# A new order of the first six steps, chunk 7 routed like the others, later transposes, and an unrolled ring of expert blocks

## The chip, the cores and the metric

The kernel runs on one core of a Trainium2 chip. The metric is the device time of one execution in microseconds; lower is better. Inputs and outputs are float32 in the chip's memory.

## The reference

Windowed attention, a two-layer network with a Mish activation, and a layer of eight experts with a skip decision for each token. Cut to what matters:

```python
attn_out = _attn_ref(q, k, v)                # 4 batches, 8 heads, 576 positions, head width 64; a query sees
                                             # the 64 positions up to its own; softmax with scale 1/8
x = attn_out.transpose(0, 2, 1, 3).reshape(2304, 512)
h = x @ w_in                                 # w_in 512 x 2048
sp = np.log1p(np.exp(np.minimum(h, 20.0)))   # h itself where h > 20
x = (h * np.tanh(sp)) @ w_out                # w_out 2048 x 512
do_compute = x @ w_skip > 0
xc = x[do_compute]
logits = xc @ w_gate                         # 8 experts
e_idx = np.argmax(logits, axis=1)
gate_w = softmax(logits)[chosen expert]
for e in range(8):                           # w1[e] 512 x 1024, w2[e] 1024 x 512
    y[e_idx == e] = gate_w * (np.maximum(xc @ w1[e], 0.0) @ w2[e])
out[do_compute] = xc + y                     # the other rows are x itself
```

## The kernel before

**Chunks and steps.** The 2304 tokens are worked in NC = 9 chunks of 256: 64 positions of each of the 4 batches. Within a chunk the hidden width 2048 is worked in NJ = 8 steps of 256 columns. Step J = 8c + j is one call of `tick(J)` on each engine. TensorE (PE) does `up(J+2)` in it, 24 matmuls that make the hidden values two steps ahead, and `down_hi(J)` and `down_lo(J)`, 8 and 4 matmuls that add step J's product to the two tiles of y. Values are split into a rounded part and a rest (hi and lo) so that three fast matmuls stand for one of full precision; the first four steps (RAW = 4) use the unsplit product instead, `down_raw`, in 8 matmuls of float32. Mish takes, for each step, on ScalarE (ACT) `mish_exp` (L977) and `mish_recip` (L984, L986), on VectorE (DVE) `mish_n` (L1252, L1257) and `mish_a`, `mish_b`, `mish_c` (L1266, L1272, L1285), on GpSimd (POOL) `mish_q` (L1701); then ACT rounds the product (`g_hi_out`, L992) and POOL takes the rest (`g_lo_out`, L1707).

**Attention** of the next chunk runs between the steps, one group of one batch for every two steps: `scores` (L606, in the steady state L627), `soften` on DVE (mask and maximum), `att_exp` on ACT, `normalise` on DVE, `probs_T` (L635), `probs_T_out` on ACT, `weigh_v` (L648), `x_hi_out` on ACT, `x_lo_out` on DVE (L1245). Chunk 0 has its own forms, `scores_first` to `x_lo_out_first` (L1201), ahead of all steps, with small dummy matmuls (`keep_warm`, L596) between them.

**Weights.** The 16 slices of the two matrices come in 512 KB loads issued by SyncE (SP, L429). Each is rounded by POOL or ACT (`round_slice`, L946 on ACT) and its rest is taken by DVE (`rest_of_slice`, L1209), in the orders HI_POOL, HI_ACT and LO_DVE. `load_group(g)` waits until the attention group two before it has been weighed, and everything behind it on SP's queue waits with it.

**Routing** of chunk c-1 is done in the steps of chunk c. y is transposed in two tiles (`y_T`, L750, copied out by ACT, L1006). For chunks 0 to 6 the logits are made in columns (`logits_columns`, L662, in step j = 2, copied by ACT, then `logits_back`, L672, in j = 4, summed by DVE, L1302); for chunks 7 and 8 they are made by rows (`logits`, L760, 8 matmuls for each tile; DVE copies them out, L1296). Then DVE's `choose` and `gate_and_row`, and a scatter by POOL. For chunk 7 these steps come one j later than for the others (`route_at`).

**Early experts.** DVE's `pick_first` (L1371 and on) at the end of step 63 and `pick_second` at the end of step 64 choose the two fullest experts from the counts of chunks 0 to 6, so that SP can load their weights (2 MB each, L476, L480) and POOL their tokens during chunk 8.

**Expert blocks.** 128 tokens of one expert are a block: `expert_up` (L822, 64 matmuls) and `expert_down` (L840, 24). Blocks 0 to 7 are written out. From block 8 on every engine runs a loop, `Fori(2, 7)`, whose body holds RING = 4 blocks, each inside an `If` on the number of blocks `nblk`, nested, so that the first false `If` skips the rest of the body. The inputs give 12 blocks, 8 to 11 in the loop's first turn. After the last block POOL scatters the rows, DVE waits for that and does one tiny instruction, and the engines meet at the end (L55).

**What sets the order.** Each engine works its own list in order; semaphores tie them. Up to step 5 (OPENING = 6) the lists of PE, ACT and DVE are written out by hand, afterwards `tick` makes them.

## Time and profile before

| | us |
|---|---|
| median of 3 runs | 689.06 (688.34 to 690.7) |
| the profiled execution | 690.12 |
| its span, first to last instruction | 688.5 |
| PE busy | 665.6 (97%), 5192 matmuls |
| DVE, ACT, POOL busy | 486.4, 360.3, 254.3 |

Waits are idle time of an engine just before an instruction, put down to what released it. A line number is that of the kernel's line or of its helper. Matmuls overlap: one of 512 columns is shown as 0.39 us long, but the next starts 0.23 us after it, so that stretches from start to start tell more than durations.

### The profile page before, as it was taken

Reading aid. Unit: us, or ns where it says so; the run is one execution under the profiler, and the core shown is the slowest. Engines: PE = TensorE matmul, PEld = TensorE weight load, DVE = VectorE, ACT = ScalarE, POOL = GpSimd, SP = SyncE. Lnnn points to the kernel's source line nnn. Section 1 sums busy time; section 2 is a strip of 40 time slices with the busy share of each in tenths; the row PEclk is TensorE's granted clock in tenths of the full one; section 3 lists DMA queues with packets and bytes.
Section 4 is the critical chain, followed back from the end, with each engine's and each line's share of the span. In section 5 each row is a group of like instructions: output and inputs, shape, how many; then the busy total and the mean of one; then the engine's idle time right before and its main releaser. Section 6 shows DMA issues by size and latency. Waiting matters only on the chain.

```text
span 688.5 us, 14197 instructions
## 1 busy us (share of the span) xinstructions
PE 665.6 (97%) x5192; PEld 581.0 (84%) x5192; DVE 486.4 (71%) x961; ACT 360.3 (52%) x791; POOL 254.3 (37%) x231
## 2 busy tenths in 40 slices
PE   7798999999999999999999999999999999999994
PEld 6676888888888888888888888888888998999994
DVE  5896777876777795786696687689589754464461
ACT  5545576555664565556556556644453243533530
POOL 4411343443352444353343345345553332221221
PEclk9999999999999999999999999999999999999998
DMA  9815131162156222134115115002658899999940
GB/s 281 276 58 164 40 95 53 39 93 62 63 92 109 77 57 83 45 88 87 40 46 132 39 40 126 14 19 45 245 167 258 258 397 393 370 340 354 354 148 2
DMA packets 62948, 97.20 MB, mean 141 GB/s; under 512 B 23126, under 2 KB 27222, under 8 KB 62880
## 3 DMA queue, kind: packets, MB, share of 16 engines
q1 hardware_dynamic: 59264, 91.01, 43.5%
q0 software_dynamic: 3168, 4.51, 2.1%
q8 instruction: 41, 0.67, 0.4%
q10 hardware_dynamic: 448, 0.79, 0.4%
q14 instruction: 27, 0.22, 0.1%
HBM read 84.97 MB, written 13.73 MB: 143 GB/s over the span
## 4 chain that ended last, share of the span: by engine, by line
PE 80%; DVE 10%; issue 4%; DMA 3%; ACT 3%; SPq 0%; DVEq 0%; POOLq 0%; ACTq 0%
PE Y L715 24%; PE H L687 16%; PE H L822 11%; PE OB L840 10%; PE PTB L687 8%; PE OB L648 3%; PE SB_ L627 2%; PE SB_ L635 2%; PE Y L729 1%; DVE a_sb L1272 1%; DVE a_sb L1266 1%; DVE g_sb L1285 1%; DVE u_sb L1252 1%; DMA wout<-moe_w_out 1%; DMA xs<-y_rows,blk_tok 1%
## 5 line engine op out<-in xcount | busy, mean ns | idle before, releaser
L1701 POOL TENSOR_TENSOR q_sb<-n_sb,r_sb 128x512 f32<-128x512 f32 x72 | 94.0, 1306 | 270.6 <-ACT r_sb L986 155.9
L715 PE MATMUL Y<-wout_hi,g_hi 128*128 128x512 f32 x272 | 111.3, 409 | 3.4 <-ACT g_hi L992 3.1
L687 PE MATMUL H<-x_hi,win_hi 128*128 128x256 f32 x384 | 111.3, 290 | 0.6 <-DVE x_lo L1201 0.5
L687 PE MATMUL H<-x_hi,win_lo 128*128 128x256 f32 x384 | 108.0, 281 | 0.0
L687 PE MATMUL H<-x_lo,win_hi 128*128 128x256 f32 x384 | 107.9, 281 | 0.0
L715 PE MATMUL Y<-wout_lo,g_hi 128*128 128x512 f32 x272 | 107.5, 395 | 0.0
L1707 POOL TENSOR_TENSOR g_lo<-g_sb,g_hi 128x512 fp32r<-128x512 f32 x68 | 88.2, 1296 | 2.4 <-ACT g_hi L992 1.9
L822 PEld LDWEIGHTS H<-xT,w 128*128 128x128 f32 x768 | 87.6, 192 | 1.0
L822 PE MATMUL H<-xT,w 128*128 128x128 f32 x768 | 88.0, 276 | 0.0
L1252 DVE TENSOR_SCALAR u_sb<-e_sb 128x512 f32<-128x512 f32 x72 | 36.5, 508 | 62.3 <-ACT e_sb L977 61.6
L687 PEld LDWEIGHTS H<-x_hi,win_hi 128*128 128x128 f32 x384 | 72.3, 188 | 5.2 <-issue 2.9
L715 PE MATMUL Y<-wout_hi,g_lo 128*128 128x512 f32 x272 | 75.1, 398 | 0.0
L992 ACT CAST g_hi<-g_sb 128x512 fp32r<-128x512 f32 x68 | 42.0, 618 | 60.6 <-DVE g_sb L1285 60.6
L687 PEld LDWEIGHTS H<-x_lo,win_hi 128*128 128x128 f32 x384 | 72.5, 189 | 1.0 <-issue 0.2
L687 PEld LDWEIGHTS H<-x_hi,win_lo 128*128 128x128 f32 x384 | 72.4, 189 | 0.0
L984 ACT ACTIVATE r_sb<-n_sb,two 128x512 f32<-128x512 f32 x72 | 52.1, 723 | 30.8 <-DVE n_sb L1257 30.4
L715 PEld LDWEIGHTS Y<-wout_hi,g_hi 128*128 128x128 f32 x272 | 51.2, 188 | 15.0 <-ACT g_hi L992 5.2
L715 PEld LDWEIGHTS Y<-wout_hi,g_lo 128*128 128x128 f32 x272 | 50.3, 188 | 11.8 <-POOL g_lo L1707 0.3
L715 PEld LDWEIGHTS Y<-wout_lo,g_hi 128*128 128x128 f32 x272 | 51.2, 188 | 9.2
L1037 ACT CAST w_hi<-w 128x1024 fp32r<-128x1024 f32 x44 | 43.1, 1045 | 24.7 <-DMA w<-moe_w 24.7
L687 PE MATMUL PTB<-x_hi,win_hi 128*128 128x256 f32 x192 | 55.4, 288 | 0.0
L1433 DVE TENSOR_TENSOR w_lo<-w,w_hi 128x1024 fp32r<-128x1024 f32 x44 | 51.4, 1223 | 4.1 <-ACT w_hi L1037 4.0
(219 smaller groups left out, 1397.8 us busy)
## 6 DMA issues: line engine op xcount, KB each, us to landing
w<-moe_w SPq DMA_DIRECT2D x23, 2048.0 KB, 10.2
kT<-k_T SPq DMA_DIRECT2D x32, 256.0 KB, 3.3
vw<-v_w SPq DMA_DIRECT2D x32, 256.0 KB, 3.2
y_rows<-ytile SPq DMA_DIRECT2D x36, 128.2 KB, 7.5
out_rows<-ytile SPq DMA_DIRECT2D x36, 128.0 KB, 2.6
win<-moe_w_in SPq DMA_DIRECT2D x8, 512.0 KB, 8.6
qbd<-q_T SPq DMA_DIRECT2D x64, 64.0 KB, 2.6
wout<-moe_w_out SPq DMA_DIRECT2D x8, 512.0 KB, 8.3
```

What stands on the lines that cost most here:

```text
L648: last = nc.tensor.matmul(OB[hp, r * W:(r + 1) * W], vw[:, b % 2, r * P + h * 64:r * P + h * 64 + 64], pT[:, i, half * 64:half * 64 + 64], ...
L687: last = nc.tensor.matmul(HM3[J % 3][:, f, :], wt[:, j, d, f * P:(f + 1) * P], xt[:, c % 2, d, :], start=(n == 0), stop=(n == 3 * DB - 1))
L715: last = nc.tensor.matmul(Y[t][:, :], gt[:, J % 2, lo:lo + P], wt[:, 2 * j + f, :], start=(j == 0 and f == 0 and wt is wout_hi and gt is g ...
L822: last = nc.tensor.matmul(H[half][:, f * P:(f + 1) * P], w1[:, par, o:o + P], xT[:, par, d, :], start=(d == 0), stop=(d == DB - 1))
L840: last = nc.tensor.matmul(OB[:, :], hT[:, f, :], wt, start=first[0], stop=(f == EFB - 1 and hT is hT_lo))
L984: nc.scalar.activation(r_sb[:, J % 2, :], n_sb[:, J % 2, :], ACT.Ln, bias=two[:, 0:1]).then_inc(t_ok, 1)
L992: nc.scalar.copy(g_hi[:, J % 2, :], g_sb[:, :]).then_inc(ghi_ok, 1)
L1037: nc.scalar.copy(w2_hi[par][:, k * 1024:(k + 1) * 1024], w2_raw(b, slot_)[:, k * 1024:(k + 1) * 1024])\
L1252: nc.vector.tensor_scalar(u_sb[:, :], e_sb[:, :], EXP10, 2.0, ALU.min, ALU.add).then_inc(u_ok, 1)
L1433: nc.vector.tensor_tensor(w2_rest(b, slot_)[:, at], w2_raw(b, slot_)[:, at], w2_hi[par][:, at].bitcast(FP32), ALU.subtract)\
L1701: nc.gpsimd.tensor_tensor(q_sb[:, :], n_sb[:, J % 2, :], r_sb[:, J % 2, :], ALU.mult).then_inc(q_ok, 1)
L1707: nc.gpsimd.tensor_tensor(g_lo[:, J % 2, :], g_sb[:, :], g_hi[:, J % 2, :].bitcast(FP32), ALU.subtract)\
```

## The change

It does five things. (1) The hand-written lists of PE, ACT and DVE up to step 5 get another order, the order of slices in LO_DVE changes a little, and PE does 36 dummy matmuls at the start in place of 28. (2) On SP, two slices go ahead of the load of attention group 6 and the last four ahead of that of group 7. (3) Chunk 7 is routed in columns like chunks 0 to 6, at the same j as they, its `logits_back` in j = 3 of chunk 8; in j = 2 there is no `weigh_v` in front of `logits_columns`. (4) For all chunks up to 7 the transposition of y's second tile moves from between `down_hi` and `down_lo` of j = 1 to behind `probs_T` of j = 2, ahead of `down_hi`, and its copy on ACT from before `g_hi_out` to behind `probs_T_out`. `pick_first`, `pick_second` and POOL's `early_tokens` each come one step later. (5) The loop over the expert blocks is written out for blocks 8 to 27 on all engines, nested `If`s on `nblk > b` with constants for b.

```diff
@@ -293,7 +293,7 @@
         HI_POOL = (0, 2, 4, 6, 8)
         HI_ACT = (10, 12, 14, 9, 11, 13, 15, 1, 3, 5, 7)
-        LO_DVE = (0, 2, 4, 6, 8, 12, 14, 10, 9, 11, 13, 15, 1, 3, 5, 7)
+        LO_DVE = (0, 2, 4, 6, 8, 12, 14, 10, 11, 13, 9, 15, 1, 3, 5, 7)
         RAW = 4
         OPENING = 6
         QUAD = 2 * NB + 1
@@ -324,16 +324,17 @@
         def route_at(c, j):
-            return None if c == 0 else j - 1 if c == NC - 1 else j
-
-        def in_columns(c):
-
-            return c < NC - 2
+            return None if c == 0 else j
         def columns_at(J):
             c, j = divmod(J, NJ)
-            return c - 1 if c > 0 and j == 2 and in_columns(c - 1) else None
+            return c - 1 if c > 0 and j == 2 else None
+
+        def back_at(J):
+
+            c, j = divmod(J, NJ)
+            return c - 1 if c > 0 and j == (3 if c == NC - 1 else 4) else None
         def x_at(J):
@@ -343,11 +344,10 @@
             for b in range(2, NE):
                 block_of(b, b // RING, b % RING)
-            with eng.Fori(NE // RING, LOOPS) as i:
-                with ExitStack() as guards:
-                    for n in range(RING):
-                        guards.enter_context(eng.If(i * RING + n < nblk))
-                        block_of(i * RING + n, i, n)
+            with ExitStack() as guards:
+                for b in range(NE, NBLK):
+                    guards.enter_context(eng.If(nblk > b))
+                    block_of(b, b // RING, b % RING)
         def third(b):
@@ -444,12 +444,12 @@
             load_group(5, 1)
             for s in (8, 3, 10, 5, 12):
                 load_slice(s)
-            load_group(6, 0)
             for s in (7, 14):
                 load_slice(s)
-            load_group(7, 1)
+            load_group(6, 0)
             for s in (9, 11, 13, 15):
                 load_slice(s)
+            load_group(7, 1)
             sp.wait_ge(consts, 2)
             sp.dma_start(wrt[:, :, 0:NE + 1], w_rt.rearrange("(d p) n -> p d n", p=P)).then_inc(wrt_in, 16)
@@ -544,11 +544,10 @@
             nblk = sp.value_load(cbi_i[0:1, NV - 1:NV], min_val=NE, max_val=NBLK)
             for b in range(EARLY + 1, NE):
                 load_block(b, b // RING, b % RING)
-            with sp.Fori(NE // RING, LOOPS) as i:
-                with ExitStack() as guards:
-                    for n in range(RING):
-                        guards.enter_context(sp.If(i * RING + n < nblk))
-                        load_block(i * RING + n, i, n)
+            with ExitStack() as guards:
+                for b in range(NE, NBLK):
+                    guards.enter_context(sp.If(nblk > b))
+                    load_block(b, b // RING, b % RING)
             sp.wait_ge(y_out[0], 128 * 6)
             sp.wait_ge(y_out[1], 128 * 5)
@@ -739,10 +738,7 @@
                 elif final:
                     pe.wait_ge(y1_ok, 1)
                 elif not final:
-                    if in_columns(c):
-                        pe.wait_ge(yT_ok, c * 2 + 1)
-                    else:
-                        pe.wait_ge(lg_ok, c * 2 + 1)
+                    pe.wait_ge(yT_ok, c * 2 + 1)
                     beside = scores_at((c + 1) * NJ + 1)
                     if beside:
                         pe.wait_ge(masked_ok, masked(beside[0] * 4 + beside[1]))
@@ -785,20 +781,16 @@
                 if gp:
                     probs_T(*gp)
                 route = route_at(c, j)
-                if route == 0:
-                    y_T(c - 1, 0)
-                if route == 2 and not in_columns(c - 1):
-                    logits(c - 1, 1)
-                if route == 4 and in_columns(c - 1):
-                    logits_back(c - 1)
+                if route in (0, 2):
+                    y_T(c - 1, route // 2)
+                if back_at(J) is not None:
+                    logits_back(back_at(J))
                 down_hi(J)
-                if route == 0 and not in_columns(c - 1):
-                    logits(c - 1, 0)
-                if route == 1:
-                    y_T(c - 1, 1)
                 down_lo(J)
                 if gp:
                     weigh_v(*gp, columns_at(J))
+                elif columns_at(J) is not None:
+                    logits_columns(columns_at(J)).then_inc(pv_ok, 1)
                 if c > 0 and j == 5:
                     ranks(c - 1)
@@ -844,7 +836,7 @@
                     last.then_inc(bz_ok, 1)
             pe.wait_ge(ones_ok, 1)
-            keep_warm(28)
+            keep_warm(36)
             scores_first(0)
             scores_first(1)
             scores_first(2)
@@ -859,35 +851,37 @@
             keep_warm(4)
             weigh_v_first(1)
             probs_T_first(3)
+            scores(1, 0)
             weigh_v_first(2)
             weigh_v_first(3)
-            scores(1, 0)
             up(0)
             up(1)
             probs_T(1, 0)
+            up(2)
             weigh_v(1, 0)
             scores(1, 1)
-            up(2)
             down_raw(0)
+            up(3)
             probs_T(1, 1)
-            up(3)
-            scores(1, 2)
             down_raw(1)
             weigh_v(1, 1)
+            scores(1, 2)
             up(4)
+            down_raw(2)
             probs_T(1, 2)
             up(5)
             weigh_v(1, 2)
-            down_raw(2)
+            up(6)
             scores(1, 3)
             down_raw(3)
-            up(6)
+            up(7)
             probs_T(1, 3)
-            up(7)
+            down_hi(4)
             scores(2, 0)
-            down(4)
             weigh_v(1, 3)
-            down(5)
+            down_lo(4)
+            down_hi(5)
+            down_lo(5)
             for J in range(OPENING, NC * NJ):
                 tick(J)
             rows_T(1, 0, 1)
@@ -1055,18 +1049,16 @@
                 if gx:
                     x_hi_out(*gx)
                 if columns_at(J - 1) is not None:
-                    logits_columns_out(columns_at(J - 1), gx[0] * 4 + gx[1])
+                    logits_columns_out(columns_at(J - 1), gx[0] * 4 + gx[1] if gx else NG)
                 if ahead:
                     mish_recip(J + 1)
                 if c > 0 and j == 0:
                     y_out_of_psum(c - 1)
-                if route_at(c, j) == 2:
-                    y_T_out(c - 1, 1)
                 g_hi_out(J)
                 if gp:
                     probs_T_out(*gp)
-                if route_at(c, j) == 0:
-                    y_T_out(c - 1, 0)
+                if route_at(c, j) in (0, 2):
+                    y_T_out(c - 1, j // 2)
                 if c > 0 and j == 4:
                     route_exp(c - 1)
                 if late_slice(J):
@@ -1093,8 +1085,8 @@
             exp_first(2)
             probs_T_out_first(0)
             exp_first(3)
+            x_hi_out_first(0)
             probs_T_out_first(1)
-            x_hi_out_first(0)
             probs_T_out_first(2)
             x_hi_out_first(1)
             probs_T_out_first(3)
@@ -1106,31 +1098,31 @@
             probs_T_out(1, 0)
             mish_exp(1)
             round_slice(10)
+            mish_recip(1)
             x_hi_out(1, 0)
-            mish_recip(1)
             round_slice(12)
             att_exp(1, 1)
             mish_exp(2)
             round_slice(14)
+            round_slice(9)
+            mish_recip(2)
+            round_slice(11)
+            mish_exp(3)
+            round_slice(13)
             probs_T_out(1, 1)
-            mish_recip(2)
-            mish_exp(3)
+            mish_recip(3)
+            x_hi_out(1, 1)
+            round_slice(15)
             att_exp(1, 2)
-            x_hi_out(1, 1)
-            mish_recip(3)
             mish_exp(4)
+            mish_recip(4)
             probs_T_out(1, 2)
-            round_slice(9)
-            round_slice(11)
             mish_exp(5)
-            mish_recip(4)
-            round_slice(13)
-            round_slice(15)
             x_hi_out(1, 2)
+            mish_exp(6)
+            mish_recip(5)
             att_exp(1, 3)
-            mish_recip(5)
             g_hi_out(4)
-            mish_exp(6)
             probs_T_out(1, 3)
             mish_recip(6)
             g_hi_out(5)
@@ -1460,12 +1452,10 @@
                     mish_n(J + 1)
                 if gp:
                     normalise(*gp)
+                if c == NC - 1 and j == 4:
+                    logits_back_out(c - 1)
                 mish_g(J)
-                if route_at(c, j) == 0 and not in_columns(c - 1):
-                    logits_out(c - 1, 0)
-                if route_at(c, j) == 2 and not in_columns(c - 1):
-                    logits_out(c - 1, 1)
-                if route_at(c, j) == 4 and in_columns(c - 1):
+                if back_at(J) is not None and c < NC - 1:
                     logits_back_out(c - 1)
                 if gx:
                     x_lo_out(*gx, columns_at(J - 1))
@@ -1479,9 +1469,9 @@
                     step, count = steps(rstep, (c - 1) * RSTEPS + 8)
                     gate_and_row(c - 1, step)
                     assert count[0] == RSTEPS - 7, count
-                if c == NC - 2 and j == 7:
+                if c == NC - 1 and j == 0:
                     pick_first()
-                if c == NC - 1 and j == 0:
+                if c == NC - 1 and j == 1:
                     pick_second()
                 if c == NC - 1 and j in (3, 5):
                     rest_of_w2(0, 0, j - 3)
@@ -1503,61 +1493,61 @@
             normalise_first(1)
             soften_first(3)
             normalise_first(2)
+            normalise_first(3)
             rest_of_slice(0)
-            normalise_first(3)
             x_lo_out_first(0)
             x_lo_out_first(1)
+            soften(1, 0)
             x_lo_out_first(2)
+            x_lo_out_first(3)
             rest_of_slice(2)
-            x_lo_out_first(3)
-            soften(1, 0)
+            normalise(1, 0)
             rest_of_slice(4)
             dve.wait_ge(consts, 2)
             mish_n(0)
-            normalise(1, 0)
             rest_of_slice(6)
-            rest_of_slice(8)
             mish_a(0)
             mish_n(1)
+            mish_b(0)
+            mish_c(0)
             soften(1, 1)
-            mish_b(0)
-            x_lo_out(1, 0)
-            mish_c(0)
+            rest_of_slice(8)
             mish_a(1)
-            rest_of_slice(12)
             normalise(1, 1)
             mish_b(1)
             mish_n(2)
+            x_lo_out(1, 0)
             mish_c(1)
+            rest_of_slice(12)
             rest_of_slice(14)
+            mish_n(3)
             mish_a(2)
             rest_of_slice(10)
             soften(1, 2)
             mish_b(2)
-            mish_n(3)
+            x_lo_out(1, 1)
             mish_c(2)
-            x_lo_out(1, 1)
             normalise(1, 2)
+            mish_n(4)
+            rest_of_slice(11)
+            rest_of_slice(13)
             mish_a(3)
-            mish_n(4)
             mish_b(3)
+            mish_c(3)
+            mish_a(4)
+            mish_b(4)
+            x_lo_out(1, 2)
+            mish_n(5)
             rest_of_slice(9)
-            rest_of_slice(11)
-            mish_c(3)
-            rest_of_slice(13)
-            x_lo_out(1, 2)
             soften(1, 3)
-            mish_a(4)
-            mish_n(5)
-            mish_b(4)
-            normalise(1, 3)
             mish_c(4)
             mish_a(5)
+            mish_b(5)
+            normalise(1, 3)
             mish_n(6)
-            mish_b(5)
             rest_of_slice(15)
+            mish_c(5)
             soften(2, 0)
-            mish_c(5)
             x_lo_out(1, 3)
             for J in range(OPENING, NC * NJ):
                 tick(J)
@@ -1759,7 +1749,7 @@
                     all_placed(c - 1)
                 if c == 1 and j == 1:
                     nc.gpsimd.memset(blank[:, :], 0.0).then_inc(blank_ok, 1)
-                if c == NC - 1 and j == 1:
+                if c == NC - 1 and j == 2:
                     early_tokens()
                 if c == NC - 1 and j == 3:
                     pool.wait_ge(g2_ok, J)
```

## Rows read from the trace of the kernel before

**Rows 1.** Page, part 1: busy time, share of the span, instructions

```profile
PE 665.6 (97%) x5192; PEld 581.0 (84%) x5192; DVE 486.4 (71%) x961; ACT 360.3 (52%) x791; POOL 254.3 (37%) x231
```

**Rows 2.** Busy time by stage: stretch, PE, PEld, DVE, ACT, POOL, clock, DMA

```profile
0.00:19.01 19.01, 14.40 (x213) 12.53 (x213) 11.13 (x31) 10.29 (x41) 8.33 (x24) 1.00 0.94 285
19.01:78.33 59.32, 53.72 (x361) 41.64 (x361) 49.26 (x73) 33.51 (x80) 15.48 (x13) 0.97 0.44 138
...
470.00:533.90 63.90, 61.17 (x394) 53.81 (x393) 51.23 (x123) 30.54 (x48) 28.52 (x27) 1.00 0.57 190
```

**Rows 3.** PE's waits over the span: total, times, longest

```profile
PE Y L729 <- DVE g_raw L1285: 3.2, 2, 1.9
PE Y L715 <- ACT g_hi L992: 3.1, 5, 1.4
```

**Rows 4.** Same view as Rows 2, of single pieces of PE's list

```profile
39.24:42.16 2.92, 2.92 (x27) 2.92 (x26) 1.68 (x3) 1.84 (x3) 0.69 (x1) 1.00 0.02 6
42.16:43.05 0.89, 0.89 (x11) 0.89 (x9) 0.89 (x1) 0.60 (x1) 0.89 (x1) 1.00 0.00 0
43.05:46.58 3.53, 3.53 (x11) 1.34 (x9) 3.50 (x5) 0.89 (x5) 0.20 (x1) 1.00 0.00 0
46.58:47.19 0.61, 0.61 (x17) 0.54 (x16) 0.58 (x2) 0.61 (x4) 0.00 (x0) 1.00 0.00 0
50.13:50.49 0.36, 0.36 (x7) 0.36 (x5) 0.36 (x1) 0.16 (x1) 0.28 (x1) 1.00 0.56 155
75.43:78.33 2.90, 2.90 (x13) 2.36 (x13) 2.31 (x6) 2.89 (x11) 1.29 (x1) 1.00 0.36 58
```

**Rows 5.** Instructions of PE in order of time, opening: start, length, idle before

```profile
33.66 5.39 PE L729 MATMUL Y<-wout,g_raw 128*128 128x512 f32 x8 [1.92 <-DVE g_raw L1285]
...
59.98 0.70 PE L729 MATMUL Y<-wout,g_raw 128*128 128x512 f32 x1 [1.27 <-DVE g_raw L1285]
```

**Rows 6.** The same of SP and of ACT

```profile
49.66 2.04 SPq L429 DMA_DIRECT2D wout<-moe_w_out  x4
...
55.67 1.04 ACT L946 CAST wout_hi<-wout 128x1024 fp32r<-128x1024 f32 x1 [4.26 <-DMA wout<-moe_w_out]
```

**Rows 7.** The same of DVE

```profile
17.38 1.24 DVE L1209 TENSOR_TENSOR win_lo<-win,win_hi 128x1024 fp32r<-128x1024 f32 x1
```

**Rows 8.** DVE's groups from 19 to 78.3: busy, mean ns, idle before

```profile
L1209 DVE TENSOR_TENSOR win_lo<-win,win_hi 128x1024 fp32r<-128x1024 f32 x6 | 9.4, 1576 | 0.0
...
L1209 DVE TENSOR_TENSOR wout_lo<-wout,wout_hi 128x1024 fp32r<-128x1024 f32 x4 | 5.1, 1284 | 5.0 <-ACT wout_hi L946 4.9
```

**Rows 9.** Instructions of PE in chunk 4, in order of time

```profile
268.81 1.17 PE L715 MATMUL Y<-wout_hi,g_lo 128*128 128x512 f32 x4
...
274.95 1.09 PE L715 MATMUL Y<-wout_hi,g_lo 128*128 128x512 f32 x4
```

**Rows 10.** Instructions of DVE and PE around chunk 8's start

```profile
467.58 2.79 DVE L1371 TENSOR_TENSOR df<-nextrow,ecap 128x8 f32<-128x8 f32 x1
...
475.87 0.50 PE L715 MATMUL Y<-wout_hi,g_hi 128*128 128x512 f32 x1 [1.43 <-ACT g_hi L992]
...
484.89 0.17 DVE L1296 COPY lg<-MB 128x9 f32<-128x9 f32 x1 [3.84 <-PE MB L760]
...
496.06 0.17 DVE L1296 COPY lg<-MB 128x9 f32<-128x9 f32 x1 [2.79 <-PE MB L760]
```

**Rows 11.** Logits by rows and in columns on PE

```profile
276.58 0.64 PE L662 MATMUL OB<-yT,wrt 128*32 128x256 f32 x8
...
483.90 0.96 PE L760 MATMUL MB<-wrt,yT 128*128 128x9 f32 x8
```

**Rows 12.** The end: chain piece (start, length), then POOL's sequencer lines (ns)

```profile
681.57 2.27 DMA out_rows<-ot,blk_tok
...
L55 POOLq DRAIN  x1: 4971/4971/4971, 683.3 to 683.3; - x1
...
L346 POOLq COMPARE_BRANCH  x5: 48/53/63, 681.4 to 683.3; - x5
```

## The prediction, made before the change was run

> **What bounds the kernel now.** I read the page's busy times first: PE is busy 97% of the span [rows 1]. DVE's 71% is an average, so I cut the span into stages. From the first `up` at 19.01 to the end of step 5's product at 78.33 PE is busy 53.72 of 59.32 us and DVE 49.26; in chunk 8 and after it, 470 to 533.9, PE is busy 61.17 of 63.90 [rows 2]. The stages between are full. So the time lies in three places only: the opening, chunk 8, and what comes after the last matmul. PE's own waits name the releasers: 3.2 us for `g_raw` in two waits and 3.1 us for `g_hi` in five [rows 3]. Elsewhere only PE's own work counts, and it changes only where matmuls are dropped or stand in another company.
>
> **The opening (part 1 and 2).** First PE's floor. One `up` takes 2.92 us, `scores` 0.89, `down_raw` 3.53, `weigh_v` 0.61, `probs_T` 0.36, a split `down` 2.90 [rows 4]. From the first `up` on, the new list holds 8 `up` (23.4), 4 `scores` (3.6), 4 `down_raw` (14.1), 4 `weigh_v` (2.4), 4 `probs_T` (1.4; I take 1.6, as the first one behind an `up` starts slowly) and 2 `down` (5.8): 50.9 us. The stretch took 59.32, so 8.4 us of it are not PE's work: 1.92 and 1.27 us stood before two `down_raw`, and behind the first of these PE ran 5.39 us for what takes 3.60 [rows 5]; the clock of this stage averages 0.97, and 0.03 of 59.3 us is the same 1.8 us: one piece ran at 1.2 GHz in place of 2.4 after PE had idled, and goes back to full rate if the idling goes.
>
> Then what made DVE late. ACT waited 4.26 us for slice 9, because SP issued the last four slices at 49.66, behind the load of group 7 [rows 6]; DVE waited 4.9 us for the rounded slices in turn [rows 8]. The change issues them ahead of that load, behind group 6's, so about 18 us earlier: this idle time goes. What is late next is DVE itself. Its busy time in the stretch, 49.26, less the 2.31 behind the last product that PE needs [rows 4], less the softening of group 4 that moves in front (about 1.4, half of a step's Mish; estimate), plus slice 2's split of 1.24 that moves in [rows 7], is 46.8. Its idle time, 59.32 - 49.26 = 10.1, less 4.9, is 5.2.
>
> The start. PE does 8 more dummies; 28 of them take some 3.3 us, so the first scores come 0.8 us later, and the chain of the first chunk behind them too. On DVE two `x_lo_out_first` now stand behind the softening of group 4, so `up(0)` starts no sooner: I take 19.7. What pays is that the softening and ACT's exponentials of group 4 are ready about 1.3 us earlier.
>
> So by PE alone the stretch ends at 19.7 + 50.9 = 70.6 (gain 7.7). By DVE it ends at 19.7 + 46.8 + 5.2, plus the last 2.9 us that are PE's: 74.6 (gain 3.7). Going through the new lists instruction by instruction with the durations of the old ones I find PE waiting some 0.9, 0.3 and 1.8 us ahead of the first three raw products, none long enough to be sure that the clock falls again, and the end at 73.6 (gain 4.7). I take 4.5. The bounds: 7.7, and 1.0 if DVE is held more often. This needs a word: six slices' splits took 1576 ns on average where 1240 is what one takes alone [rows 7, 8], since a DVE instruction with two SBUF inputs that meets a POOL operation lasts until that one is over. Such holds are 6 us of DVE's 49.26. Their number depends on which instructions meet, which I can't foresee.
>
> **The early steps of chunk 1.** The late slices are rounded there, and `g_hi` is just late in j = 2. ACT's copy of y's second tile leaves the front of that `g_hi_out`, but DVE was the later one: 0.2 us (0 to 0.6).
>
> **The transposition (part 4).** In chunk 4 `down_lo` behind a transposition took 1.17 us, behind other products 1.09 [rows 9]. Moved next to `probs_T`, where the switch to transposes is paid anyway, it costs PE nothing more and saves that 0.08: 7 chunks, 0.6 us. It adds 0.36 us before `down_hi` of j = 2, but PE comes there 0.4 us earlier. The copy on ACT now delays the next `mish_exp` by some 0.1 us; the `g_hi` of j = 3 had 1.0 us to spare, so nothing (if that cover is gone, 0.1 a chunk). Bounds 0 and 0.7.
>
> **Chunk 8 (parts 3 and 4).** The first small instruction of `pick_first`, on 8 columns, took 2.79 us, held by two POOL operations in a row. `mish_n(65)` was queued behind it, then ACT's reciprocal, the copies of y and `g_hi(64)`: PE waited 1.43 us [rows 10]. Without it `g_hi(64)` comes 1.1 to 1.4 us earlier, and y's own copy ends about when PE arrives: this stop goes. The picks now sit in the slack of steps 64 and 65. I expect each to be held once by a `mish_q` or `g_lo_out` (1.3 us each) and PE to wait about 0.45 us behind each: 0.9 back. The logits by rows go: two times 8 matmuls of 0.96 us as shown, against one of 0.64 and a short way back [rows 11], about 0.9 us of PE's time. With them go two waits of DVE, 3.84 and 2.79 us, for PE's logits [rows 10]. But in j = 3 ACT now waits for the columns, then rounds expert weights, and DVE takes their rests before it turns to `mish_n(69)`: PE waits there about 1.1 us instead of 0.56. From j = 5 on the ACT and DVE chain is the bound, not PE, so what PE's list lost is not earned in full. Step 70's `down_hi` I find at 514.5 in place of 515.9: 1.4 us gained. Bounds 0 and 3.3 (all waits for `g_hi`). Choosing later delays SP's load of expert weights and POOL's of tokens by 2 to 6 us: the tokens are gathered 13 us later, but the first weight load ends about when ACT wants it; if it is late, 1 us, inside these bounds.
>
> **The unrolled ring (part 5).** The blocks themselves are PE-bound and keep their 13.1 us each. Behind the last scatter POOL makes five turns through the loop's branches, 681.4 to 683.3, and only then its DRAIN, 4.97 us long, ends the span; the scatter's own transfer had landed 2.27 us after its start, at 683.8 [rows 12]. If the drain takes 4.97 us from its start, 1.9 us are to be had; if it waits for something behind the landing, nothing. A branch now leads over 16 written-out blocks, to code that may have to be fetched; the nearest price is a trip to memory and back such as those 2.27 us: the tail can then lie 0.4 us later than before. I take 0.4 us gained, between 1.9 gained and 0.4 lost.
> The Trainium skill, page "Runtime: NRT & Kernel Launch", section "Instruction fetch mechanics", says that a taken branch whose target is outside the two pages at hand stalls for a fetch. By this rule the one long branch costs and the four short ones it replaces did not, which is the lost end; the trace of before has no such long branch on POOL, so it can't show it.
>
> **The sum.** 4.5 + 0.2 + 0.6 + 1.4 + 0.4 = 7.1 us off the profiled 690.12 (span 688.5, 1.6 around it), 683.0. The profiled execution lay 1.06 above the median of 689.06: 682.0.
>
> **The rivals.**
> A. DVE stays the bound of the opening: its holds and waits are those of before but for the late slices, and chunk 8 gives nothing. For it speaks that DVE is busy 83% of the stretch, and that a searched order is as fragile as its durations. Gain 2 to 4: about 686.
> B. The lists go through without a stop, the picks find gaps, the drain moves: 7.7 + 0.6 + 0.6 + 3.3 + 1.9 = 14 at most; some 11 is plausible: 678.
> C. Nothing to measure: the opening's gain is lost to its later start and one more spell at half clock (1.8), chunk 8's to holds of the picks. 688 to 690.
> D. Slower: in the opening POOL's eight `mish_q` and `g_lo_out` (1.3 us each, 10.3 in all) each meet a DVE instruction of two SBUF inputs. Place: DVE between 20 and 70 us. Holds double from 6 to 12 us and DVE keeps its 10.1 us of idle time, since each hold also delays ACT: the stretch ends 6 us later instead of 4.5 earlier, and the whole is 6 - 2.6 = 3.4 slower, 692.5. It decides from holds of 8.6 us on. Against it: before, about half of those eight met such an instruction, and the idle time behind the late slices goes in any case.
> E. The long branch costs more than thought, 3 us on POOL: 684.5, inside the range.
>
> **How the numbers follow.** Forecast (4 to 10 us gained) 0.60, with E in it; A 0.17; B 0.07; C 0.10; D 0.06. About 2 us, 0.3%, is what a measurement can tell from no change. Faster by more: 0.84; within: 0.10; slower: 0.06. The range leaves out C, D and the far half of B: 677.5 to 686.8. It takes in the opening's bound by DVE and chunk 8 without gain.
>
> **What would show it.** After: step 6 (the `up` into PTB that follows step 5's `down_lo`) starts near 73.6 instead of 78.33; no ACT wait for `moe_w_out` above 1 us; the 5.39 us `down_raw` is 3.6 long and the half-clock spell is gone; L1209 and L1266 still show means well above 1240 and 680 ns; `down_lo` is nowhere 1.17 in chunks 2 to 7 behind `down_hi`; the small instruction of L1371 is at step 64, and the wait of 1.43 us before `down_hi(64)` is gone; L1296 appears only for chunk 8; PE's last `down_lo` lies near 517; POOL's DRAIN starts 1 to 2 us after the last scatter's issue. I am wrong if the opening's gain is below 3 us with the late slices in time (then DVE's holds are the bound), if a new wait over 1.5 us stands at a pick, or if the drain's end stays 4.5 us behind the landing (then part 5 is worth nothing).

## The result, and the profile after the change

Median 682.32 us (681.1 to 682.52, three runs) against 689.06: a ratio of 0.9895 [0.9868, 0.9921], 6.7 us. The profiled execution is the median one: 682.32, span 680.6 against 688.5, so 7.9 us of span went between the two profiles.

The page's part 1 and the stages as in [rows 1, 2], from the first `up` to step 6's first `up`, and then 63.5 us from step 63's `down_lo` ([rows 2] has 63.9 us there, from 0.4 us ahead of that `down_lo`); the columns are stretch, PE, PEld, DVE, ACT, POOL, clock, DMA:

```profile
PE 662.3 (97%) x5194; PEld 579.4 (85%) x5194; DVE 484.2 (71%) x960; ACT 361.4 (53%) x792; POOL 252.8 (37%) x230
...
19.17:72.43 53.26, 51.35 (x361) 41.14 (x361) 47.68 (x73) 33.24 (x79) 14.32 (x13) 1.00 0.49 158
464.60:528.10 63.50, 61.18 (x400) 53.70 (x400) 53.31 (x131) 31.06 (x49) 28.18 (x27) 1.00 0.59 201
```

The first stretch took 59.32 us before and takes 53.26, its clock is 1.00 where it was 0.97, and DVE idles 5.6 us of it where it idled 10.1. PE's waits over the span, where [rows 3] had 3.2 us for `g_raw` and 3.1 for `g_hi`:

```profile
PE Y L714 <- ACT g_hi L986: 2.6, 3, 1.6
...
PE OB L647 <- ACT pT L956: 1.1, 1, 1.1
PE H L686 <- DVE x_lo L1193: 1.1, 1, 1.1
PE SB_ L801 <- DMA xs<-y_rows,blk_tok: 0.9, 1, 0.9
PE Y L728 <- DVE g_raw L1277: 0.8, 2, 0.6
```

Where the 7.9 us went is read best from the starts of `down_lo`, one in each step, which bound the same work in every kernel. With it stand two variants of the experiments, and the end of PE's work:

```
                             before   after   opening_only  chunk8_only
start to down_lo(7)           90.70   84.60       85.19        92.58
down_lo(7) to (15), chunk 1   55.39   55.45       55.41        55.41
(15) to (63), chunks 2 to 7  324.30  324.52      324.28       324.36
(63) to (71), chunk 8         53.90   52.40       53.97        52.70
(71) to PE's end, blocks     155.46  155.69      156.10       156.84
PE's end to the span's end     8.79    7.95        8.79         8.79
```

The opening gave 6.1 us, chunk 8 1.5, the tail 0.8; chunks 1 to 7 and the blocks took 0.5 back. How well such pieces repeat can be read from the other profiles. Chunk 8 repeats within 0.1 us: 53.90 to 53.99 in the four kernels with the old one (before, `opening_only`, `slices_only`, `ring_only`), 52.40 to 52.46 in the five with the new one (after, `warm28`, `drain_late`, `pT_early`, `best`). The opening doesn't: `down_lo(7)` starts at 90.55 to 92.58 in the four with the old lists and loads (before, `ring_only`, `chunk8_only`, `later_only`), at 84.44 to 86.71 in the five with the new ones (after, `opening_only`, `spread`, `drain_late`, `picks_early`). The two groups lie far apart, but the 6.1 us is the difference of two single executions; the groups' means differ by 6.4.

**The opening.** PE and ACT in order of time, columns start, length, idle before. The raw product that ran 5.39 us [rows 5] takes its normal length, no wait of PE in this stretch is over 1.1 us, and ACT waits 1.92 us for slice 9 where it waited 4.26 [rows 6]:

```profile
30.71 3.70 PE L728 MATMUL Y<-wout,g_raw 128*128 128x512 f32 x8 [0.62 <-DVE g_raw L1277]
...
37.53 3.64 PE L728 MATMUL Y<-wout,g_raw 128*128 128x512 f32 x8
42.26 0.69 PE L647 MATMUL OB<-pT,vw 128*64 128x64 f32 x16 [1.09 <-ACT pT L956]
...
47.06 3.70 PE L728 MATMUL Y<-wout,g_raw 128*128 128x512 f32 x8 [0.20 <-DVE g_raw L1277]
```

```profile
37.01 1.05 ACT L940 CAST wout_hi<-wout 128x1024 fp32r<-128x1024 f32 x1 [1.92 <-DMA wout<-moe_w_out]
```

DVE's groups from 19.17 to 72.43, as [rows 8]. The wait of 4.9 us is gone, and the splits of `win`'s slices last 1270 ns on average where they lasted 1576:

```profile
L1201 DVE TENSOR_TENSOR win_lo<-win,win_hi 128x1024 fp32r<-128x1024 f32 x7 | 8.8, 1270 | 0.0
...
L1201 DVE TENSOR_TENSOR wout_lo<-wout,wout_hi 128x1024 fp32r<-128x1024 f32 x4 | 4.8, 1218 | 0.0
```

**Chunk 8.** PE's waits of 1.43, 0.56 and 0.57 us are two now. First DVE, then PE, then ACT and DVE ahead of PE's wait:

```profile
467.51 0.86 DVE L1363 TENSOR_TENSOR df<-nextrow,ecap 128x8 f32<-128x8 f32 x1
...
468.57 1.27 DVE L1367 TENSOR_SCALAR taken<-df 128x8 f32<-128x8 f32 x1
...
475.07 1.05 DVE L1351 TENSOR_SCALAR ohe<-rev,turn 128x8 f32<-128x8 f32 x1
```

```profile
495.01 0.50 PE L714 MATMUL Y<-wout_hi,g_hi 128*128 128x512 f32 x1 [1.64 <-ACT g_hi L986]
...
508.65 0.50 PE L714 MATMUL Y<-wout_hi,g_hi 128*128 128x512 f32 x1 [0.58 <-ACT g_hi L986]
```

```profile
487.08 2.00 ACT L1031 CAST w_hi<-w 128x1024 fp32r<-128x1024 f32 x2 [0.37 <-DMA w<-moe_w]
...
488.16 2.89 DVE L1425 TENSOR_TENSOR w_lo<-w,w_hi 128x1024 fp32r<-128x1024 f32 x2 [2.69 <-ACT w_hi L1031]
490.97 0.41 DVE L1244 TENSOR_SCALAR u_sb<-e_sb 128x512 f32<-128x512 f32 x1
```

The picks' small instructions are held three times (0.86, 1.27, 1.05 us) and PE waits behind none of them. It waits at step 68: ACT rounds two quarters of expert weights, DVE stands 2.69 us for them, splits both, and only then takes up the Mish of step 69.

**The tail.** The last piece of the chain of waits, then the sequencers' lines (ns) that answer to [rows 12]:

```profile
674.37 2.55 DMA out_rows<-ot,blk_tok
...
L55 POOLq DRAIN  x1: 5741/5741/5741, 674.6 to 674.6; - x1
...
L349 PEldq COMPARE_BRANCH  x1: 3742/3742/3742, 668.3 to 668.3; - x1
L349 DVEq COMPARE_BRANCH  x1: 67/67/67, 672.8 to 672.8; - x1
```

The drain starts 0.26 us after the scatter's start where it started 1.77 after it, but is 5.74 us long in place of 4.97.

### The profile page after: what moved, and what is told of

Its sections match the earlier page's. It is cut to its first block, busy times and chain, and to the rows that moved or that the text cites. A ratio compares the mean times of both kernels' runs of the same rounds, so it can differ in the third digit from the quotient of the medians.

```text
span 680.6 us, 14026 instructions
## 1 busy us (share of the span) xinstructions
PE 662.3 (97%) x5194; PEld 579.4 (85%) x5194; DVE 484.2 (71%) x960; ACT 361.4 (53%) x792; POOL 252.8 (37%) x230
## 4 chain that ended last, share of the span: by engine, by line
PE 83%; DVE 7%; DMA 3%; issue 3%; ACT 2%; SPq 0%; DVEq 0%; POOLq 0%; ACTq 0%
PE Y L714 24%; PE H L686 17%; PE H L814 11%; PE OB L832 10%; PE PTB L686 9%; PE OB L647 3%; PE SB_ L626 2%; PE SB_ L634 2%; DMA w<-moe_w 1%; PE Y L728 1%; DMA xs<-y_rows,blk_tok 1%; DVE a_sb L1264 1%; PE MB L746 1%; DMA wout<-moe_w_out 1%; DVE g_sb L1277 1%
```

## The experiments

Each ratio is taken against runs of the kernel before that were made beside the experiment. Their medians were 690.07 us (25 runs) for `opening_only`, `slices_only`, `ring_only` and `chunk8_only`, 688.99 (7 runs) for `warm28` and `spread`, and 688.94 (11 runs) for `pT_early` and `best`.

**The opening alone, and of it the order of loads alone.** `opening_only` is the kernel before with parts 1 and 2 (the lists, LO_DVE, the dummies, SP's order); `slices_only` has SP's order alone:

```diff
-            load_group(6, 0)
             for s in (7, 14):
                 load_slice(s)
-            load_group(7, 1)
+            load_group(6, 0)
             for s in (9, 11, 13, 15):
                 load_slice(s)
+            load_group(7, 1)
```

> The kernel before with parts 1 and 2 alone: the new lists of PE, ACT and DVE up to step 5, the new slice order, 36 dummies, and the last slices' loads ahead of the groups' loads. In the profile of the whole change step 6's first up starts at 72.4 us instead of 78.3. If the opening is independent of the rest, it does so here too, and the time falls by 5.9 us less nothing: ratio 0.9915. Rival: what is won in the opening is given back in chunk 1, where DVE and ACT take the late slices: then the gain at the start of chunk 2 is below 5 us.

Measured: 684.6 us, ratio 0.9906 [0.9878, 0.9935], 5.5 us by the medians. `down_lo(7)` starts at 85.19, also 5.5 us earlier than in the profile of before, and chunk 8 takes 53.97 us, as before: what the opening gives is given back nowhere.

> The kernel before with SP's order alone: two slices loaded ahead of attention group 6, four ahead of group 7, every list else as before. Theory 1 (the late load was the cause of the stops at 55 to 60 us): ACT's wait of 4.26 us for slice 9 goes, the down_raw of step 3 starts about 3 us sooner, and half of the opening's 5.9 us is earned by this alone. Theory 2 (the lists are the cause, the load only the last to arrive): under 1.5 us are gained, since the next thing, the Mish chain behind DVE's splits, is as late.

Measured: 686.89 us, ratio 0.9961 [0.9943, 0.9979], 3.2 us by the medians; `down_lo(7)` at 88.04, 2.66 us earlier than in before and 2.5 to 4.5 earlier than in the four profiles with the old opening. ACT no longer waits for slice 9. PE in order of time, first raw product:

```profile
33.77 5.40 PE L729 MATMUL Y<-wout,g_raw 128*128 128x512 f32 x8 [1.92 <-DVE g_raw L1285]
...
43.17 3.60 PE L729 MATMUL Y<-wout,g_raw 128*128 128x512 f32 x8
```

The wait of 1.27 us at 59.98 [rows 5] is gone, the 1.92 us and the half clock behind it stay. So of the opening's 5.5 us about half comes from the loads (2.7 by the profiles, 3.2 by the medians) and the rest from the new lists, under which that one wait and its spell are gone. Which of the edits in the lists of PE, ACT and DVE takes the wait away was not separated. By the code, the new lists can't run without the new loads: `weigh_v(1, 1)`, which is group 5, would wait through ACT's list for the rounding of slice 9, whose load stands on SP's queue behind that of group 7, and this waits for that same `weigh_v`. No run shows it.

**The ring alone.** `ring_only` is the kernel before with part 5:

```diff
-            with eng.Fori(NE // RING, LOOPS) as i:
...
+                for b in range(NE, NBLK):
+                    guards.enter_context(eng.If(nblk > b))
+                    block_of(b, b // RING, b % RING)
```

> The kernel before with part 5 alone: blocks 8 to 27 written out. In the whole change the end came 7.8 us after DVE's last gating operation began, where it was 8.5 before: 0.7 us gained, with POOL's DRAIN starting 0.3 us after the last scatter's start, not 1.8. If that is the unrolling's own, it shows here as 0.6 to 0.8 us between that operation and the span's end, and nothing else changes; in time it can't be told from no change. Rival: the 0.7 us are the scatter of that execution; then this run shows 8.5 again.

Measured: 689.18 us, ratio 0.9981 [0.9958, 1.0004]. The scatter starts at 683.29; the drain:

```profile
L55 POOLq DRAIN  x1: 5739/5739/5739, 683.5 to 683.5; - x1
```

Its end is 6.0 us behind the scatter's start, against 6.74 before; from PE's end to the span's end it takes 7.95 us, as in the changed kernel. So the 0.8 us are the ring's own. `drain_late` asks what the length means: the changed kernel, where POOL waits for the last rows to land before it goes to the end.

```diff
             blocks(pool, nblk, expert_block)
+            pool.wait_ge(o_out, 12 * 16)
```

> The changed kernel with one wait more: POOL waits for the last scatter's rows to land before its DRAIN. In all five profiles the drain's end lay 4.97 us behind the later of two points: its own start, and the end of POOL's 1.0 us for the scatter. Theory 1 (the drain has its own length, from POOL being free): it now starts at the landing, 2.3 to 2.6 us after the scatter's start, is 4.97 long, and the span's end moves 1.3 to 1.6 us back, to 7.3 to 7.6 us after the scatter's start, where it was 6.2. Theory 2 (it waits for something of the transfer): it gets shorter by as much as it starts later, and the end stays 6.2 us after the scatter's start.

Measured, in a single run of 685.12 us: scatter from 675.83 to landing at 678.11, then

```profile
L55 POOLq DRAIN  x1: 4975/4975/4975, 678.3 to 678.3; - x1
```

A drain with nothing left to wait for still takes 4.97 us, as theory 1 has it. In all thirteen profiles it ends 4.97 to 4.99 us after the later of its own start and the end of POOL's scatter instruction (1.02 us long, to 675.39 in the changed kernel; + 4.97 is 680.36, and it ends within 0.02 of that). So the five turns cost only what lay behind the scatter's own 1.0 us: 0.8, not 1.9.

**Chunk 8 and the transposition alone.** `chunk8_only` is the kernel before with parts 3 and 4; `later_only` of these only the choices and the early tokens one step later, routing of chunk 7 by rows kept:

```diff
-                if c == NC - 2 and j == 7:
+                if c == NC - 1 and j == 0:
                     pick_first()
-                if c == NC - 1 and j == 0:
+                if c == NC - 1 and j == 1:
                     pick_second()
```

> The kernel before with parts 3 and 4 alone: chunk 7 in columns, y's second tile transposed behind the probabilities, picks and early tokens a step later. From the profile of the whole change: 1.5 us gained between the down_lo of step 63 and that of step 71, nothing in chunks 1 to 7 (where I had forecast 0.6), a wait of 1.6 us before the down_hi of step 68. Time ratio 0.998. Rival: the 1.5 us depend on the shift of the DMA by the earlier opening; then less than 1 us or more than 2 us here.

> The kernel before with the choice of the early experts alone a step later, and POOL's loads of their tokens with it; routing and transposes as before. The prediction's step: the wait of 1.43 us before step 64's down_hi is the choice's, held 2.8 us by POOL. Then it goes here, and about 1.1 us are gained between the down_lo of step 63 and that of step 64; by step 71 between 0.5 and 1.1 remain. Rival: the routing in columns is what saved the time; then nothing is gained by step 71, since the logits by rows still hold DVE.

`chunk8_only` gave 688.98 us, ratio 0.999 [0.9963, 1.0017]; chunk 8 takes 52.70 us in it, 1.3 less than in `opening_only`. A gain of this size is under what ten runs of this kernel resolve, and is read from the steps. `later_only` gave 691.39 in a single run, with two spells at half clock in it (6.83 and 3.41 us), so that its time is not compared. Steps 64 to 71, from `down_lo` to `down_lo`:

```
step           64    65    66    67    68    69    70    71    sum
before        7.44  6.88  6.50  6.61  6.45  6.29  7.35  6.37  53.89
after         6.18  5.99  6.07  6.62  7.54  6.27  7.35  6.37  52.39
chunk8_only   6.17  5.97  6.06  6.62  7.87  6.28  7.35  6.37  52.69
later_only    5.89  7.07  8.02  6.61  6.66  6.27  7.36  6.37  54.25
picks_early   7.46  5.90  6.08  6.62  7.56  6.29  7.33  6.37  53.61
spread        6.19  5.98  6.08  6.62  7.02  7.25  6.52  6.84  52.50
```

Moved alone, the choice makes step 64 shorter by 1.55 us and step 66 longer by 1.52, with the wait now in front of step 66:

```profile
489.10 0.50 PE L715 MATMUL Y<-wout_hi,g_hi 128*128 128x512 f32 x1 [1.69 <-ACT g_hi L992]
...
502.73 0.50 PE L715 MATMUL Y<-wout_hi,g_hi 128*128 128x512 f32 x1 [0.77 <-ACT g_hi L992]
```

`picks_early` is the reverse, the changed kernel with the choices where they were (POOL's early tokens stay late):

> The changed kernel with the two choices of an expert back in the steps of the kernel before (the first in chunk 7's last step, the second in chunk 8's first), everything else as changed. If the later choice is what took the waits of the first three steps of chunk 8, they come back: steps 63 and 64 take 7.1 to 7.5 and 6.5 to 7.0 us instead of 6.8 and 6.18, and the eight steps of chunk 8 take 53.2 to 53.9 us instead of 52.39. If routing in columns took them, the eight steps take 52.4 to 52.8 us and the wait of 1.6 us ahead of the third part of step 68 goes or shrinks under 1 us, since nothing of a choice is queued in front of its operand.

Measured, in a single run: 682.51 us; step 64 takes 7.46 us again, with a wait in front of the first transposition of y, for ACT's copy:

```profile
469.36 0.66 PE L746 MATMUL MB<-ident,ytile 128*128 128x128 f32 x4 [0.92 <-ACT ytile L994]
...
496.04 0.51 PE L714 MATMUL Y<-wout_hi,g_hi 128*128 128x512 f32 x1 [1.66 <-ACT g_hi L986]
```

So neither of the two edits gives chunk 8's gain alone: in columns (with the moved transpositions) and with the early choice the chunk takes 53.6 us, by rows with the late one 54.25, with both 52.4. The wait at step 68 is there with either choice, so it doesn't come from the picks. Of the 1.2 us by which this chunk is longer in `picks_early` the end shows only 0.3: it had reached step 63 0.2 us sooner, and its blocks took 154.93 us where the changed kernel's took 155.69. The blocks' difference is near the wait of 0.85 us for `xs` ahead of a block, which `picks_early` doesn't have. The later choice doesn't by itself make that wait: `spread`, `warm28`, `drain_late`, `pT_early` and `best` have the later choice and no such wait, and before, with the early one, has one of 0.61.

**Step 68's wait.** `spread` is the changed kernel with the second weights of expert 0 rounded and split one quarter a step, steps 67 to 70, instead of two in 67 and two in 69:

```diff
-                if c == NC - 1 and j in (3, 5):
-                    rest_of_w2(0, 0, j - 3)
-                    rest_of_w2(0, 0, j - 2)
+                if c == NC - 1 and 3 <= j <= 6:
+                    rest_of_w2(0, 0, j - 3)
```

> The changed kernel with the first expert's second weights rounded and split one quarter a step in j = 3, 4, 5, 6 of chunk 8, not two in j = 3 and two in j = 5. In the changed kernel PE waits 1.64 us before step 68's down_hi and 0.58 before step 70's. Theory 1 (two quarters in one step make ACT and DVE late): the first wait falls to under 0.5 us, and step 71's down_lo comes 1 to 2 us sooner. Theory 2 (the wait comes from the late arrival of the weights after the later choice, and from DVE being held by POOL): it stays above 1.2 us, or moves to step 69.

Measured: 681.46 us, ratio 0.9889 [0.9866, 0.9912]; PE in chunk 8:

```profile
494.20 0.51 PE L714 MATMUL Y<-wout_hi,g_hi 128*128 128x512 f32 x1 [1.12 <-ACT g_hi L986]
...
501.45 0.51 PE L714 MATMUL Y<-wout_hi,g_hi 128*128 128x512 f32 x1 [0.91 <-ACT g_hi L986]
```

1.64 us became 1.12 and 0.91, and the chunk's sum 52.50 where it was 52.39. Theory 1 fails: two quarters in one step are not the cause alone, and dividing the work in other portions moves the wait. I take it that the whole queue of Mish and weights on ACT and DVE sets these steps; no run took work out of it.

**The start of the opening.** `warm28` is the changed kernel with `keep_warm(28)` for `keep_warm(36)`.

> The changed kernel with 28 dummy matmuls at the start, as before, and all else changed. Theory 1 (the eight more dummies only delay the first scores, 5.2 us instead of 4.6): everything up to the first up comes about 0.6 us sooner, at 18.6 in place of 19.2, and the time falls by 0.6. Theory 2 (the start is bound elsewhere, by the arrival of the values and weights that POOL rounds): under 0.2 us.

Measured: 682.6 us, ratio 0.9904 [0.9867, 0.9941], no gain that can be told. The first `up` starts at 18.02, 1.15 us sooner, `down_lo(7)` at 85.53, 0.9 later. PE waits longer for the probabilities' copy, and then the clock falls (stretches of PE's time, columns as above):

```profile
42.04 0.90 PE L647 MATMUL OB<-pT,vw 128*64 128x64 f32 x16 [1.95 <-ACT pT L956]
```

```profile
42.30:44.00 1.70, 1.70 (x21) 1.58 (x16) 1.19 (x2) 1.67 (x4) 0.00 (x0) 0.51 0.00 0
44.00:45.90 1.90, 1.90 (x11) 1.90 (x11) 0.88 (x2) 0.48 (x1) 0.00 (x0) 0.54 0.50 86
45.90:47.50 1.60, 1.60 (x16) 1.60 (x15) 1.60 (x4) 1.06 (x5) 0.35 (x1) 1.00 0.98 312
```

The granted clock is at 1.2 GHz for 3.41 us. (The next expectation speaks of 7.1 us at half the clock; that is the length of a whole stretch in which the clock averages 0.76. The spell is 3.41 us long and costs 1.7.) `drain_late`'s profile has the same, at 44.81 behind a wait of 1.86 us, and its `down_lo(7)` starts at 86.71.

`pT_early` moves that copy ahead of a rounding in ACT's list; `best` has it and `keep_warm(28)`:

```diff
             mish_exp(3)
+            probs_T_out(1, 1)
             round_slice(13)
-            probs_T_out(1, 1)
```

> The changed kernel, with the copy of the four transposed probability tiles of group 7's second half (0.59 us on ScalarE at 41.62) one place ahead of the rounding of slice 13 (1.04 us). In the changed kernel TensorE waits 1.09 us for that copy at 42.26, and in two executions of its variants a wait of 1.86 and 1.95 us at this place was followed by 7.1 us at half the clock. Theory 1 (the wait is the copy's place in ScalarE's list): the copy ends about 0.94 us sooner, the wait shrinks from 1.09 us to between 0 and 0.3 us, no half-clock stretch follows in the opening, step 6 starts 0.5 to 0.9 us sooner (71.6 to 71.9 instead of 72.43), and the median is 681.4 to 681.9. Theory 2 (the stretch behind is set by VectorE and ScalarE, and they get done no sooner): the wait reappears in front of the next raw matmuls, step 6 starts at 72.4 as before, the time is that of the changed kernel, 682.3.

> The copy of the probabilities ahead of slice 13's rounding, as in the run before it, and 28 matmuls of the warm-up in place of 36 (at full speed 8 of them are 0.8 to 1.15 us). Theory 1: the fewer warm-up matmuls brought the first up 1.15 us sooner and lost it only to a half-clock stretch behind the wait for that copy; with that wait gone both are kept, step 6 starts at 70.6 to 71.2 and the median is 680.3 to 680.9. Theory 2: the middle of the opening is bound by ScalarE's and VectorE's lists or by the loads of w_out's slices, not by when TensorE begins: the first up is 1.15 us sooner, the waits behind it grow by as much, and the time is 682.0 to 682.6.

`pT_early`: 681.74 us (680.63 to 682.28, six runs), ratio 0.9889 [0.9861, 0.9917]. The median lies where theory 1 had it, but the wait didn't shrink in the profile and step 6 starts at 72.58, so that neither theory holds as a whole. PE, then ACT:

```profile
41.92 0.69 PE L647 MATMUL OB<-pT,vw 128*64 128x64 f32 x16 [1.48 <-ACT pT L956]
...
47.22 3.70 PE L728 MATMUL Y<-wout,g_raw 128*128 128x512 f32 x8 [0.69 <-DVE g_raw L1277]
```

```profile
37.63 1.05 ACT L940 CAST wout_hi<-wout 128x1024 fp32r<-128x1024 f32 x1 [3.26 <-DMA wout<-moe_w_out]
...
41.29 0.58 ACT L956 COPY pT<-SB_ 128x512 f32<-128x512 f32 x1
```

From slice 9's rounding to the copy's end it is 4.24 us where it was 5.20, as meant; but the slice landed 0.6 us later, PE got there 0.7 us sooner, and the wait is 1.48. What sets this place is the landing of slice 9: in the six profiles with ACT's list as in the changed kernel this matmul starts 5.25 to 5.27 us after it, and in `pT_early` 4.32. In `best`'s profile it landed at 36.05, and PE went through:

```profile
40.51 0.69 PE L647 MATMUL OB<-pT,vw 128*64 128x64 f32 x16
...
45.88 3.70 PE L728 MATMUL Y<-wout,g_raw 128*128 128x512 f32 x8 [0.76 <-DVE g_raw L1277]
...
561.54 0.77 PE L832 MATMUL OB<-w_hi,hT_hi 128*128 128x512 f32 x1 [1.76 <-DVE hT_lo L1436]
```

There `down_lo(7)` starts at 83.39, 1.2 us ahead of the changed kernel; but a wait of 1.76 us in the blocks, with a spell of 3.41 us at half clock behind it, took more than that, and this execution took 683.85. The six runs: 679.49, 680.58, 681.03, 681.45, 683.85, 684.64; median 681.24, ratio 0.9888 [0.9855, 0.992], between the ranges of the two theories. The last two are the ones with a lower mean clock, 0.994 against 0.996 to 0.997, which one more spell of this length would make. It is the lowest time seen, but its interval covers that of the changed kernel, so it can't be called faster.

## Why the prediction was right, step by step

The time was 682.32, 682.0 had been foretold. The largest term is right in its reason; that the time is right within 0.3 us is partly that errors cancel.

**The opening: 4.5 forecast, 5.9 measured** (step 6's first `up` at 72.43 for 78.33; with steps 6 and 7 6.1; by the medians of `opening_only` 5.5). The cause held: the late slices (2.7 us by `slices_only`) and the half-clock spell, which goes if its wait goes. The size was short. The first `up` starts at 19.17, not 19.7, so the start was overpriced by 0.5. The waits worked out ahead of the first three raw products, 0.9, 0.3 and 1.8, were 0.62, none and 0.20, with 1.09 ahead of `weigh_v`, where I had none. And the splits of slices averaged 1270 ns, not 1576: DVE was held 3.1 us in the stretch where it had been held 6.0 (each instruction's excess over the shortest of its form, five and nine of them). I had kept the holds of before as a constant. They go with the order, and vary within it: 5.3 to 6.1 us in the five profiles with DVE's old list, 3.1 to 4.5 in the eight with its new one, of which this execution was near the best. The bounds, 1.0 and 7.7, held it. Rival A failed by this: DVE's idle time went from 10.1 to 5.6 us, as the sum had it (5.2), and its busy time fell too. Two of the signs named for this stretch did not come: ACT's wait for slice 9 is 1.92 us, not under 1, and the means of the splits (1270) and of `mish_a` (754, L1258 now) are close to the 1240 and 680 ns of undisturbed ones, not well above.

**Chunk 1's early steps: 0.2 forecast, nothing.** 55.39 and 55.45 us.

**The transposition: 0.6 forecast, nothing.** `down_lo` is 1.09 at j = 1 now, as foretold: in chunks 2 to 7 that step fell from 7.41 to 7.05 and the next rose from 6.14 to 6.50. The four more transposes next to `probs_T`, in chunk 4:

```profile
252.70 0.60 PE L634 MATMUL SB_<-ident,pr 128*128 128x128 f32 x4
253.14 0.60 PE L746 MATMUL MB<-ident,ytile 128*128 128x128 f32 x4
253.52 0.50 PE L714 MATMUL Y<-wout_hi,g_hi 128*128 128x512 f32 x1
```

From start to start they cost 0.44 and 0.38. The error is the term "costs PE nothing more": I priced them at the 0.36 of a group that stands alone, and took the 0.08 at `down_lo` for a saving; 0.82 for the group of eight is 0.10 above twice 0.36, so that as much is paid there.

**Chunk 8: 1.4 forecast, 1.5 measured,** by other steps. The stop at step 64 went, as said. The two waits of 0.45 behind the picks did not come, though the picks were held; the wait at step 68 is 1.64 where I had 1.1. `picks_early` and `later_only` show that both edits are needed, which the prediction's sum, adding them as if each stood alone, doesn't say.

**The ring: 0.4 forecast, 0.8 measured.** Neither end was right. The drain's 4.97 us count from the end of POOL's scatter instruction, not from the landing (the loss end) and not from its own start (1.9). Nor did the sign come that DRAIN starts 1 to 2 us after the scatter; it starts 0.26 after it. The long branch, rival E: with the pause until the next instruction it took 0.5 us on POOL and 0.6 on DVE, on PE 3.74 us (3.31 in `ring_only`). PE's own short branches in the loop of before:

```profile
L346 PEldq COMPARE_BRANCH  x5: 83/214/238, 675.5 to 678.5; - x5
```

The rule of the Trainium skill, page "Runtime: NRT & Kernel Launch", section "Instruction fetch mechanics", is that a taken branch to a target out of the pages at hand stalls for a fetch. PE's 3.74 us against 0.24 at most agrees with it; POOL's branch took 0.055 us, no more than a short one [rows 12], and the next sequencer instruction came 0.43 us later where it had come 0.03 later, so that no stall of PE's size shows there. That any of this was a fetch is my reading, no run separates it. It costs nothing here since PE's sequencer meets the branch at 668.3, ahead of the last products' end at 672.66.

**Profile against median.** I had taken 1.06 us off, since the profiled execution before lay above its median. The one after did not: it is the median. The profiled times differ by 7.8 us (7.1 forecast), the medians by 6.7, so 0.7 too little in the sum and 1.06 too much for this offset cancel.

## What to carry to other kernels

A load that is late in an ordered queue can be worth moving on its own: SP's order alone gave about half of the opening's gain, and by the code the new lists depend on it. Where one engine's list is the bound over a stretch, an edit that takes a stop away is priced by the next stop in the same list, which needs the whole list walked: `later_only` and `spread` moved theirs by 13 and 7 us and gained nothing in the chunk. A saving of 0.08 us a time at one place has to be looked for at the place where the work goes.

## What the runs showed of the hardware

- POOL's drain at the program's end takes 4.97 us even when all transfers have landed (`drain_late`). It ends 4.97 to 4.99 us after the end of POOL's last indirect transfer instruction or after its own start, whichever is later, in all thirteen profiles.
- One false branch over 16 written-out blocks took PE's sequencer 3.31 to 3.89 us in the eight profiles that have it, POOL's and DVE's under 0.1, with 0.4 to 0.5 until their next instruction (but 0.12 on POOL in `drain_late`).
- Eight of the thirteen profiles have a spell at 1.2 GHz, 3.41 us long, ahead of the last products, and each of these begins about when a wait of PE of 1.76 to 2.4 us ends or within 1.5 us of it (two, `ring_only` and `later_only`, have one of 6.83 us near 15 us as well, during the dummies and chunk 0's attention). None of the spells of 3.41 us stood behind waits up to 1.69 us, nor behind two of 1.97 and 1.98 in `chunk8_only`, so a long wait brings it often, not always. Each costs 1.7 us, and a kernel with waits near that size scatters by at least as much: `best` fell into 679.5 to 681.5 at a mean clock of 0.996 to 0.997 and 683.9 to 684.6 at 0.994.
- The landing of slice 9 moved by 1.55 us between `best` and `pT_early` (36.05 and 37.60), though SP issued it within 0.15 us of the same time; PE waits 1.5 us in the one and not at all in the other. From issue to landing it took 5.3 to 7.0 us in the eight profiles with the new opening.
